# Relu rows of the second mixture's blocks: transposed by DMA as 16-bit planes in place of TensorE

## What is computed

```python
# stage 1: attention in chunks of 64 tokens -> x of 2304 tokens x 512
# stage 2: four dense experts
for e in range(4):
    h = np.maximum(x @ w1[e], 0.0)            # 512 -> 1024
    out += p[:, e:e + 1] * (h @ w2[e])        # 1024 -> 512
# stage 3: eight experts, each token goes to the one with the largest logit
expert_idx = np.argmax(x @ w_gate, axis=1)
for e in range(8):
    xe = x[expert_idx == e]
    h = np.maximum(xe @ w1[e], 0.0)
    out[mask] = gate_w[mask, None] * (h @ w2[e])
```

## Time and profile before

| | us |
|---|---|
| median of three runs (1139.31 to 1141.04) | 1140.25 |
| the profiled execution's own time | 1140.44 |
| its span, first to last instruction | 1138.7 |
| TensorE busy | 1125.5 (99%) |
| VectorE busy | 512.3 (45%) |
| ScalarE busy | 289.2 (25%) |
| GpSimd busy | 312.2 (27%) |
| 16 DMA engines, both dynamic queues | 24.9% |

### The profile page before, as it was taken

How to read it: one execution, slowest core, us unless ns; L and a number is a source line. 1 busy time by engine, 2 the same in 40 slices (tenths; PEclk the granted TensorE clock), 3 DMA queues, 4 the chain that set the end, 5 groups by cost and what they waited for, 6 DMA issues and landing times.

```text
span 1138.7 us, 19676 instructions
## 1 busy us (share of the span) xinstructions
PE 1125.5 (99%) x6886; PEld 988.1 (87%) x6887; DVE 512.3 (45%) x1142; ACT 289.2 (25%) x428; POOL 312.2 (27%) x191
## 2 busy tenths in 40 slices
PE   8999999999999999999999999999999999999996
PEld 6899888999999999999999998889877888888885
DVE  5445434322222232222223248888655545545554
ACT  3444344331111133111113311112333032032230
POOL 7300000250000024000002401100287677077591
PEclk9999999999999999999999999999999999999998
DMA  9332221420000021000002101101662662063540
GB/s 354 79 102 83 74 74 28 151 73 0 0 0 0 0 86 61 0 0 0 0 0 92 56 28 29 21 6 28 196 175 66 172 235 99 6 230 110 178 155 26
DMA packets 64725, 87.50 MB, mean 77 GB/s; under 512 B 23983, under 2 KB 48687, under 8 KB 64562
## 3 DMA queue, kind: packets, MB, share of 16 engines
q1 hardware_dynamic: 60050, 75.45, 21.6%
q0 software_dynamic: 4496, 11.56, 3.3%
q10 hardware_dynamic: 144, 0.04, 0.0%
HBM read 73.48 MB, written 10.92 MB: 74 GB/s over the span
## 4 chain that ended last, share of the span: by engine, by line
PE 96%; DMA 1%; DVE 1%; issue 0%; SPq 0%; ACT 0%; POOL 0%; DVEq 0%; POOLq 0%
PE psum L1340 15%; PE psum L1342 15%; PE psum L1341 15%; PE psum L1386 12%; PE psum L1388 11%; PE psum L1387 11%; PE psum L1574 4%; PE psum L1576 4%; PE psum L1575 4%; PE psum L1558 2%; PE psum L1268 1%; PE psum L1252 1%; PE psum L1535 1%; DMA rows<-x_rows,meta 1%; PE psum L1503 1%
## 5 line engine op out<-in xcount | busy, mean ns | idle before, releaser
L466 POOL TENSOR_TENSOR weights_r<-weights,weights_r 128x1024 fp32r<-128x1024 f32 x96 | 232.8, 2451 | 611.0 <-ACT weights_r L655 609.7
L1340 PE MATMUL psum<-xhi,weights_r 128*128 128x384 f32 (+1 forms) x772 | 260.0, 337 | 0.0
L1342 PE MATMUL psum<-xhi,weights_r 128*128 128x384 f32 (+1 forms) x772 | 257.9, 334 | 0.0
L1341 PE MATMUL psum<-xlo,weights_r 128*128 128x384 f32 (+1 forms) x772 | 257.7, 334 | 0.0
L1386 PE MATMUL psum<-weights_r,hhi 128*128 128x512 f32 x576 | 226.9, 394 | 0.0
L1388 PE MATMUL psum<-weights_r,hlo 128*128 128x512 f32 x576 | 224.8, 390 | 0.0
L1387 PE MATMUL psum<-weights_r,hhi 128*128 128x512 f32 x576 | 224.7, 390 | 0.0
L650 ACT ACTIVATE hhi<-psum 128x384 fp32r<-128x384 f32 x192 | 94.5, 492 | 481.3 <-PE psum L1342 481.3
L872 DVE SCALAR_TENSOR_TENSOR hlo<-psum,hhi 128x384 fp32r<-128x384 f32 x192 | 106.5, 557 | 219.2 <-ACT hhi L650 219.2
L1340 PEld LDWEIGHTS psum<-xhi,weights_r 128*128 128x128 f32 x772 | 144.9, 188 | 1.8
L1341 PEld LDWEIGHTS psum<-xlo,weights_r 128*128 128x128 f32 x772 | 145.0, 188 | 0.9
(11 more groups left out here) (183 smaller groups left out, 1070.7 us busy)
## 6 DMA issues: line engine op xcount, KB each, us to landing
weights<-in_moe_w SPq DMA_DIRECT2D x96, 512.0 KB, 5.7
qkT<-in_qk SPq DMA_DIRECT2D x18, 512.0 KB, 4.1
v_rows<-in_v SPq DMA_DIRECT2D x18, 256.0 KB, 3.2
x_rows<-xfin SPq DMA_DIRECT2D x18, 256.0 KB, 4.9
wg_row<-in_gate_rows SPq DMA_DIRECT2D x1, 2048.0 KB, 7.5
meta<-slot_table SPq DMA_DIRECT2D x26, 1.0 KB, 2.1
rows<-x_rows,meta POOLq DMA_INDIRECT x26, 3.9
out<-rows,meta POOLq DMA_INDIRECT x22
```

Source lines behind the costliest of these rows:

```text
L466: gp.tensor_tensor(rounded(set_, 1, c), raw(set_, c), rounded(set_, 0, c).bitcast(F32), ALU.subtract).then_inc(sem("w_lo"), 1)
L1340: mm(out_, ahi, bhi, start=(i == 0), stop=False)
L1341: mm(out_, ahi, blo, start=False, stop=False)
L1342: last = mm(out_, alo, bhi, start=False, stop=(i == n - 1))
```

## The change

- From block 2 on, TensorE no longer transposes the hidden rows. VectorE parts each raw half (no Relu yet) from PSUM into two planes of 16-bit halves (`part_h`), SyncE issues one DMA transpose for each half (`turn_h`), VectorE joins the turned planes to 32-bit words, applies Relu and writes them into PSUM banks 3 and 4 (`join_h`), and splits both halves at once into `hThi` and `hTlo` (`split_h`).
- VectorE's `take_rows` and the tile `xs` are gone. TensorE transposes straight from `rows[:, b]`, waits itself for the gathers, and its loops over blocks are unrolled so that b is a constant.
- The weight loads of places 2 to 7 move from SyncE to ScalarE's queue, ahead of the roundings of the same four chunks.
- SyncE's loop transposes for all blocks 2 to 24, the ones that are not real too.

```diff
+    h_planes = [tile(f"h_planes{i}", [P, 2, F // 2], U16, at["acc"] + 4 * NB * D + 2 * F * i) for i in range(2)]
+    h_planes_T = [tile(f"h_planes_T{i}", [P, 2, F // 2], U16, at["xfin"] + 2 * F * i) for i in range(2)]
+    h_row_T = tile("h_row_T", [P, F // 2], F32, at["xfin"] + 4 * F)
...
 sync:
-            sp.wait_ge(sem("table_ready"), 1)
-            with sp.Fori(1, E2 // 2) as half:
...
+            def turn_h(b, i):
+                sp.wait_ge(sem("hrow_ready"), seq(b) * 2 + i + 1)
+                if b > 2:
+                    sp.wait_ge(h_planes_in[i], 16 * (b - 2))
+                sp.dma_start_transpose(h_planes_T[i][:, :, :].rearrange("p h (r t) -> p (h r) t", t=P),
+                                       h_planes[i][:, :, :].rearrange("p h n -> p (h n)")).then_inc(h_planes_in[i], 16)
+            for b in range(2, NB):
+                for i in range(2):
+                    turn_h(b, i)
...
 scalar:
+            act.wait_ge(sem("table_ready"), 1)
             with act.Fori(1, E2 // 2) as half:
...
+                    for i, products in enumerate(("l1b_psum", "l2_psum")):
+                        act.wait_ge(sem("w_lo"), split[i])
+                        act.sem_inc(sem("split_seen"), 1)
+                        act.wait_ge(sem(products), through)
+                        for c in range(i * NW // 2, (i + 1) * NW // 2):
+                            act.dma_start(raw(1 - u, c), source(v1, v2, source_e, c)).then_inc(raw_in[1 - u][c], 16)
+                        for c in range(i * NW // 2, (i + 1) * NW // 2):
+                            split_hi(1 - u, e0 // 2 + (1 if u == 0 else E1 + 1), c)
...
 vector:
-            def take_rows(b):
-                vec.reduce_max(xs[:, :], rows_flat[:, ds(b * D, D)].unsqueeze(2), axis=X).then_inc(sem("xs_ready"), 1)
+            def part_h(b, i):
+                dve.wait_ge(sem("l1b_psum" if i else "l1a_psum"), seq(b) + 1 + i)
+                words = psum[:, A2_B + i, :].bitcast(U16)
+                vec.tensor_copy(h_planes[i][:, :, :], words.rearrange("p (n h) -> p h n", h=2))\
+                    .then_inc(sem("hrow_ready"), 1)
+            def join_h(b, i):
+                n = seq(b) * 2 + i - 5
+                dve.wait_ge(h_planes_in[i], (seq(b) - 2) * 16)
+                words = h_row_T[:, :].bitcast(U16)
+                then(vec.reduce_max(words.rearrange("p (n h) -> p h n", h=2), h_planes_T[i][:, :, :].unsqueeze(3), axis=X),
+                     "h_joined", n)
+                then(vec.tensor_scalar(psum[:, HT_B + i, :], h_row_T[:, :], 0.0, None, ALU.max), "h_turned", n)
+            def split_h(b):
+                n = seq(b) * 2
+                src = psum[:, HT_B:HT_B + 2, :].rearrange("x b (r t) -> x (b r) t", t=P)
+                dve.wait_ge(sem("l2_psum"), seq(b) + 1)
+                dve.wait_ge(sem("h_turned"), n - 4)
+                ins = vec.tensor_copy(hThi_r[:, :, :], src)
+                ins.then_inc(sem("hThi_ready"), 2)
+                dve.wait_ge(sem("hThi_ready"), n + 2)
+                vec.tensor_tensor(hTlo_r[:, :, :], src, hThi[:, :, :], ALU.subtract).then_inc(sem("hT_ready"), 2)
             def block_step(b):
-                take_h(b + 1)
+                part_h(b + 1, 0)
+                part_h(b + 1, 1)
                 take_xT(b + 2)
-                take_rows(b + 3)
+                join_h(b + 1, 0)
+                join_h(b + 1, 1)
                 take_result(b)
-                take_hT(b + 1)
+                split_h(b + 1)
             def spare_step(b, ahead):
                 with dve.If(real > b + 1):
-                    take_h(b + 1)
+                    part_h(b + 1, 0)
+                    part_h(b + 1, 1)
                 with dve.Else():
+                    dve.wait_ge(sem("hT_ready"), seq(b) * 2 + 2)
                     dve.sem_inc(sem("hrow_ready"), 2)
...
-                    take_hT(b + 1, [0])
+                    join_h(b + 1, 0)
+                    join_h(b + 1, 1)
                     take_result(b)
-                    take_hT(b + 1, [1])
+                    split_h(b + 1)
...
 tensor:
             def transpose_rows(b):
-                pe.wait_ge(sem("xs_ready"), seq(b) + 1)
+                n = next(n for n, batch in enumerate(BATCH) if b in batch)
+                pe.wait_ge(rows_in[n], 16 * len(BATCH[n]))
+                pe.wait_ge(sem("xT_ready"), seq(b))
...
                 second_product(b)
-                transpose_h(b + 1)
-
-            with pe.Fori(1, NR - 1) as b:
+
+            for b in range(1, NR - 1):
                 block_step(b)
...
                     first_product(b + 1)
-                    second_product(b, range(0, FT // 2))
-                    transpose_h(b + 1, halves=[0])
-                    second_product(b, range(FT // 2, FT))
-                    transpose_h(b + 1, halves=[1])
+                    second_product(b)
```

More of the change, by code:

```diff
@@ L237, in chunked_attention_then_two_moes @@
     planes_in = [sem(f"planes_in{i}") for i in range(2)]
+    h_planes_in = [sem(f"h_planes_in{i}") for i in range(2)]
     raw_in = [[sem(f"raw_in{i}_{c}") for c in range(NW)] for i in range(2)]
@@ L418, in _ @@
                     sp.dma_start(meta[:, b, :], token_of[ds(r, P), :]).then_inc(meta_in[n], 16)
-            sp.wait_ge(sem("table_ready"), 1)
-            with sp.Fori(1, E2 // 2) as half:
[L421 to L433, removed]
+            def turn_h(b, i):
[7 more added lines that the diff above has]
+                    turn_h(b, i)
+            for i in range(2):
+                sp.wait_ge(h_planes_in[i], 16 * (NB - 2))
         @block.gpsimd
@@ L775, in _ @@
                 for u in range(2):
-                    for c in range(NW):
-                        split_hi(1 - u, e0 // 2 + (1 if u == 0 else E1 + 1), c)
-            act.wait_ge(sem("table_ready"), 1)
+                    e = e0 + u
+                    source_e = act.value_load(final_expert_at[0:1, ds(e, 1)], min_val=0, max_val=E2 - 1)
+                    done = act.value_load(tab[0:1, ds(TAB_CUM + e - 2, 1)], min_val=0, max_val=NB)
+                    through, split = act.snap(done + 2), [act.snap(NW * (E1 + e - 2) + NW // 2 * (i + 1)) for i in range(2)]
+                    for i, products in enumerate(("l1b_psum", "l2_psum")):
[6 more added lines that the diff above has]
+                            split_hi(1 - u, e0 // 2 + (1 if u == 0 else E1 + 1), c)
             real = act.value_load(tab[0:1, TAB_CUM + E2 - 1:TAB_CUM + E2], min_val=NR, max_val=NB)
@@ L1173, in _ @@
             take_ahead_hTlo(1, 1)
-            rows_arrive(1)
-            take_rows(1)
             take_xT(1)
-            rows_arrive(2)
-            take_rows(2)
             take_h(1)
             take_xT(2)
-            take_rows(3)
             take_result(XB)
@@ L1185, in block_step @@
             def block_step(b):
-                take_h(b + 1)
+                part_h(b + 1, 0)
+                part_h(b + 1, 1)
                 take_xT(b + 2)
-                take_rows(b + 3)
+                join_h(b + 1, 0)
+                join_h(b + 1, 1)
                 take_result(b)
-                take_hT(b + 1)
[L1192 to L1198, removed]
+                split_h(b + 1)
+            with dve.Fori(1, NR - 1) as b:
+                block_step(b)
             real = dve.value_load(tab[0:1, TAB_CUM + E2 - 1:TAB_CUM + E2], min_val=NR, max_val=NB)
@@ L1226, in spare_step @@
                     dve.sem_inc(sem("hT_ready"), 2)
-            with dve.Fori(NR - 1, NB - 3) as b:
-                spare_step(b, 3)
-            spare_step(NB - 3, 2)
-            spare_step(NB - 2, 1)
+            with dve.Fori(NR - 1, NB - 2) as b:
+                spare_step(b, True)
+            spare_step(NB - 2, False)
             with dve.If(real > NB - 1):
@@ L1626, in spare_step @@
                         skip_second(b)
-                    pe.wait_ge(sem("hT_ready"), seq(b) * 2 + 2)
-                    pe.sem_inc(sem("hT_psum"), 2)
-            with pe.Fori(NR - 1, NB - 2) as b:
+            for b in range(NR - 1, NB - 2):
                 transpose_rows(b + 2)
```

10 lines of the change are left out of this document (2 added, 8 removed).

## The result

The changed kernel takes 1200.3 us (median of four runs, 1199.4 to 1202.8) beside 1140.2 of the kernel before on the same chip: ratio 1.0531, 95% interval 1.0513 to 1.0549. The forecast was 1132.5, with a range up to 1146. The profiled execution has a span of 1198.7 us, 60.0 more than before.

The account below looks back on a forecast made before the run. TensorE, busy 99% of the span, was taken as the bound. The terms -17.4 + 1.1 + 4.5 + 3.0 + 1.0 = -7.8 us, from 1140.44, gave 1132.6, stated as 1132.5; range 1126 to 1146.

Parts of the forecast that it names:

- TensorE's part: Block loop: removing 8 transposes from each of blocks 2 to 21 saves 17.4 us; block period 11.42 us, from 12.29.
- Weight loads beside transposes: Transposes amid weight loads: only 3 of the 12 load groups stall TensorE, 1.5 us each, 4.5 us in all.
- L: Landing time of the second half's transpose: 3.1 to 7.0 us amid loads; TensorE waits only above about 5.4.
- The new round trip: Hidden rows by DMA transpose in each block: split by 15.3 us, wanted at 17.35, slack 2.1 us.
- VectorE's part: VectorE's passes per block: 10.7 us of the 11.42 us period, so they fit with 0.7 to spare.
- VectorE becomes the bound: Rival, block loop: dearer half-word passes make VectorE's work 12.4 us a block, +7.3 us, 1147.8; chance 0.17.
- Start: SyncE's slot-table loads delay block 2's transposes, which leave at 885.7 and 886.9; cost 1.1 us.
- Last block: `split_h(21)` must wait for `second_product(20)`, so the last second product starts 4.3 us after TensorE is free; cost 3.0 us.
- End: SyncE still turns blocks 22 to 24 after the last real one; between 0 and 2 us, taken as 1.
- Weights on ScalarE, unrolling, `take_rows`: Loads issued by ScalarE and unrolled loops cost 0 us; removing `take_rows` frees some 0.1 us, left out.
- every group of loads delays a transpose: Rival, transposes amid weight loads: 12 stalls of 1.5 us in place of 3 add 13.5 us, 1146; chance 0.19.

Follow-up runs that it names:

- e1: Changed kernel with each weight chunk's load cut to 16 rows of one slice and the splits reading another tile; ratio 1.0117 to the kernel before.
- e4: As e1, with the join also leaving out the lower 16 bits (one plane joined); ratio 0.9922 to the kernel before.
- e7: Changed kernel with full weight traffic, joining only one of the two planes; ratio 1.0202 to the kernel before.
- e2: Kernel before with all of the change except the DMA transposes: loads on ScalarE, TensorE unrolled and reading `rows` directly, `take_rows` gone; ratio 0.9998.
- e3: Kernel before with only the weight loads moved to ScalarE; ratio 0.9995 to the kernel before.
- e14: Changed kernel with hidden rows made one block further ahead, three plane tiles, only real blocks turned, join and split through PSUM; ratio 1.0097 to the kernel before.
- e9: Changed kernel with joined words read directly instead of through PSUM, each half going into `hThi` and `hTlo` by itself; ratio 1.0448 to the kernel before.

## Why the prediction was wrong

- **TensorE's part** was right: no groups of 8 behind block 1, 11.36 us a block where nothing is late, against 11.42.
- **Weight loads beside transposes** is the step that failed: "only 3" groups, "3 x 1.5 = 4.5 us". Of the 54.9 us of waits in 15 places, 33.1 us in five places stand behind transposes that landed beside loads, a mean of 6.6. Three errors are in it. L was bounded by the gather's 7.0, but the second transpose of these five pairs landed after 9.0 to 13.3 us (issued at 960, 1014, 1058, 1092 and 1138), and beside gathers, which the step had left out, after up to 10.4. The count asked which groups are released by the same event; in fact ends overlap as well, and stores stretch it too. And each stall was priced by itself.
- **The new round trip** had the chain behind the landing at 2.0 + 0.7 + 2.4 = 5.1 us; it measured 5.9 to 6.1. By that TensorE waits once L is above about 4.5, and not 5.4 (an estimate, with the forecast's other terms).
- **VectorE's part** was right pass by pass (1.22, 1.32, 0.70, 1.22) and wrong as a test. "It fits, with 0.7 to spare" compared passes with the period. Late once, the round holds the landing too, 11.99 us, so that delays are kept and added to; the 2.1 us of slack are used once, not in every block. This is the second step that failed. `e1` shows it by itself (12.0 us a block in quiet stretches), and `e4` and `e7` measure it: 1.2 us less of round, 22 and 34 us less of time. The rival *VectorE becomes the bound* had the place, with another mechanism: no pass was dear.
- **The clock** stood nowhere in the working. Behind the long waits the granted clock fell (0.78 over the 8 us behind the last one, 0.50 in its slow part) and matmuls came 0.43 us apart for 3.1 to 6.1 us. TensorE's other instructions took 19.5 us more than before, some 16 of them there.
- **Start**: forecast 1.1 us, measured 2.9. The transposes of block 2 left as forecast (886.0 and 887.4 against 885.7 and 886.9), but the second landed 4.4 us later beside gathers, and not 3.1.
- **Last block**: forecast 4.3 us behind, measured 4.65. **End**: forecast 1, measured 3.2, since SyncE's queue had six transposes left at 1179.4 and they ran 17 us.
- **Weights on ScalarE, unrolling, `take_rows`**: nothing, as said (`e2`, `e3`). One wait of 2.7 us for low parts appeared.
- The rival *every group of loads delays a transpose* had the right cause and too small a size: 12 stalls of 1.5 us, instead of five behind loads with a mean of 6.6, ten more of other kinds, and a slow clock behind the nine longest.

## What to carry to other kernels

A transfer put on the critical path must be priced by what it takes amid all other traffic of its stretch, loads, gathers and stores, and not by its time alone: here 3.1 us alone and up to 13.3. When a round trip enters an engine's round, compare the round with its waits, in the late state, with the period: if it doesn't then fit, slack is used up once and every later delay adds. The cure was lead and buffers (a block more and a third tile, with only real blocks turned, took 49 us off). Even so, moving 17 us of work from the bound engine bought nothing: in `e14` TensorE still waits 26.4 us, and 13.0 of them are for weights, which the lead made the next thing to be late.

## What the runs showed of the hardware

- A transpose of 128x1024 half-words lands after 3.0 to 3.2 us alone, 3.5 to 6.1 beside stores, 3.2 to 10.4 beside gathers and 4 to 13.3 beside weight loads of up to 2 MB on another queue; the loads are slowed too (four landed after 13.6 us in the median there). Its issue took up to 5.1 us instead of 1.23.
- VectorE's `tensor_scalar` over 128x512 words from SBUF to SBUF takes 0.42 us alone, and up to 10.2 beside GpSimd's passes (`e9`); from SBUF to PSUM it takes 0.69 to 0.70 in all 40 passes of the changed kernel, beside GpSimd or not. The joining pass, from SBUF to SBUF too, is never held up (1.29 to 1.35 us in `e9`).
- Passes over 16-bit halves cost what passes over as many words cost: 1.22 us for 1024, 1.32 for the joining one, which writes every second half-word.
- The same kernel took 1.2% longer on other chips, where TensorE waited for instructions beside the gathers.
